# A table of differences made by TensorE, an earlier third weight, and last columns kept by ScalarE

## The reference

```python
# attention, for each step t of S=768 (B=2, H=8, D=40)
m_new = max(f[t] + m, i[t]); fs = exp(f[t] + m - m_new); is_ = exp(i[t] - m_new); m = m_new
C = fs * C + is_ * outer(v[t], k[t]);  n = fs * n + is_ * k[t]
y[t] = sigmoid(o[t]) * (C @ q[t]) / max(|n . q[t]|, 1)
# x: (1536, 320)
xn = x / sqrt(mean(x*x) + 1e-6) * rms_g
x  = (silu(xn @ w_gate) * (xn @ w_val)) @ w_out      # d_ff 1536
h  = x @ w_in;  out = max(0.01 * h, h) @ w_out2      # d_ff 2048
```

## Time and profile before

| what | us |
|---|---|
| median of 3 runs (lowest, highest) | 440.17 (439.88, 440.44) |
| the profiled execution | 440.19 |
| its span, first to last instruction | 438.5 |
| TensorE matmul busy | 429.8 |
| VectorE / ScalarE / GpSimd busy | 226.3 / 193.3 / 91.0 |

### The profile page before, as it was taken

One profiled execution on the slowest core, in us unless ns is written; L12 is line 12 of the kernel. 1 busy time (PEld: TensorE's weight loads), 2 busy tenths in 40 slices (PEclk: granted clock), 3 DMA queues, 4 the chain that ended last, 5 costly groups with the idle time before them and its releaser, 6 DMA issues.

```text
span 438.5 us, 8229 instructions
## 1 busy us (share of the span) xinstructions
PE 429.8 (98%) x3237; PEld 377.7 (86%) x3237; DVE 226.3 (52%) x439; ACT 193.3 (44%) x428; POOL 91.0 (21%) x97
## 2 busy tenths in 40 slices
PE   7999999999999999999999999999999999999997
PEld 5889999999788888878888888989999999999996
DVE  8856656775466555456433335353333333533534
ACT  4867753665262535235333226553343343333332
POOL 1798852212111111002333004430000000000000
PEclk9999999999999999999999999999999999999999
DMA  7887623431202410001222102300000000100101
GB/s 213 279 294 257 215 86 124 126 121 51 78 27 98 131 47 0 1 1 33 66 67 66 34 1 67 100 0 1 0 1 0 1 1 1 44 17 0 61 0 60
DMA packets 10692, 30.42 MB, mean 69 GB/s; under 512 B 1296, under 2 KB 3264, under 8 KB 10656
## 3 DMA queue, kind: packets, MB, share of 16 engines
q1 hardware_dynamic: 10656, 29.92, 21.4%
HBM read 27.90 MB, written 2.01 MB: 68 GB/s over the span
## 4 chain that ended last, share of the span: by engine, by line
PE 82%; issue 6%; POOL 4%; DMA 4%; DVE 3%; ACT 1%; SPq 0%; POOLq 0%; DVEq 0%
PE gate_ps L1166 22%; PE value_ps L1166 22%; PE out_ps L1243 9%; PE out_ps L1205 9%; PE turn_ps L1243 6%; PE out_ps L1209 3%; PE c_ps L1243 3%; PE turn_ps L1131 3%; POOL w_sb L483 2%; DMA raw<-in_w 2%; PE turn_ps L1092 1%; DMA att_sb<-in_tok 1%; PE turn_ps L1109 1%; PE c_ps L1121 1%; DMA y_acc<-in_first_gates 1%
## 5 line engine op out<-in xcount | busy, mean ns | idle before, releaser
L1166 PE MATMUL value_ps<-x_hi,w_sb 128*128 128x512 f32 (+1 forms) x280 | 68.6, 367 | 0.5 <-DVE h_lo L929 0.5
L1166 PE MATMUL gate_ps<-x_hi,w_sb 128*128 128x512 f32 (+1 forms) x280 | 68.8, 368 | 0.2
L1166 PEld LDWEIGHTS gate_ps<-x_hi,w_sb 128*128 128x128 f32 x280 | 47.4, 191 | 8.2 <-DVE x_odd L895 1.1
L1166 PEld LDWEIGHTS value_ps<-x_hi,w_sb 128*128 128x128 f32 x280 | 47.7, 191 | 7.4 <-DVE h_lo L929 0.7
L908 DVE SCALAR_TENSOR_TENSOR act_buf<-act_buf,gate_ps 128x512 f32<-128x512 f32 (+1 forms) x46 | 26.2, 569 | 48.1 <-ACT act_buf L619 47.9
L934 DVE TENSOR_TENSOR h_lo<-hid,h_hi 128x512 fp32r<-128x512 f32 x48 | 33.2, 692 | 33.7 <-ACT h_hi L638 33.7
L633 ACT ACTIVATE h_hi<-value_ps 128x512 fp32r<-128x512 f32 (+1 forms) x46 | 23.0, 500 | 58.4 <-DVE value_ps L915 58.2
L1205 PE MATMUL out_ps<-h_hi,w_sb 128*128 128x512 f32 (+1 forms) x184 | 48.2, 348 | 0.0
L638 ACT ACTIVATE h_hi<-hid 128x512 fp32r<-128x512 f32 x48 | 30.3, 632 | 37.6 <-DVE hid L922 36.5
L619 ACT ACTIVATE act_buf<-gate_ps 128x512 f32<-128x512 f32 (+1 forms) x46 | 23.1, 501 | 49.3 <-PE gate_ps L1166 49.1
L1243 PE MATMUL out_ps<-w_sb,h_hi 128*128 128x320 f32 x192 | 43.0, 309 | 0.2 <-DVE h_lo L934 0.2
(11 more groups left out here) (148 smaller groups left out, 797.5 us busy)
## 6 DMA issues: line engine op xcount, KB each, us to landing
raw<-in_w SPq DMA_DIRECT2D x12, 544.0 KB, 4.6
att_sb<-in_tok SPq DMA_DIRECT2D x12, 484.0 KB, 4.8
raw<-in_w SPq DMA_DIRECT2D x16, 352.0 KB, 3.0
expo<-decay_scratch SPq DMA_DIRECT2D x10, 512.0 KB, 5.3
att_sb<-in_qk SPq DMA_DIRECT2D x24, 160.0 KB
out_y<-y_acc SPq DMA_DIRECT2D x12, 160.0 KB, 1.9
consts_sb<-in_consts SPq DMA_DIRECT2D x1, 129.5 KB, 2.7
y_acc<-in_first_gates SPq DMA_DIRECT2D x1, 112.0 KB, 2.6
```

Source lines behind the costliest of these rows:

```text
L1166: last = nc.tensor.matmul(ps[:, 0:n], lhs, rhs, start=(j == 0), stop=(j == len(xs) - 1))
```

## The change

There are four edits. (1) The later input gates stay as they are; in place of five transposes of the subtracted table TensorE makes ten matmuls that accumulate in pairs, the gates' block against a unit matrix of 16 x 16 and the block of `stab` against the same with -1, which ScalarE writes once into a new tile `minus_unit` from the constants. The subtraction at L968 and the wait for it go. (2) For tile 1 ScalarE, not VectorE, copies the last columns, one half after each of its exponential groups; the semaphore `first_kept` becomes one for each tile. (3) ScalarE rounds weight 2 ahead of `square(0)`, not behind it. (4) SyncE issues the load of weight 2 ahead of its wait for the sums and their store, not behind them.

```diff
--- before.py
+++ after.py
@@ -141,7 +141,9 @@
 
             unit = sb(first, "unit", [P, P], BF16)
             unseen = sb(first, "unseen", [P, P], BF16)
-            used = 4 * (2 * ATT + EXPO * H * P + 2 * H * DV + 6 * DM + 16 + 2 * H + 2 * PAIRS * DV + 3 * TILES * H
+
+            minus_unit = sb(first, "minus_unit", [P, NG])
+            used = 4 * (2 * ATT + EXPO * H * P + 2 * H * DV + 6 * DM + 16 + NG + 2 * H + 2 * PAIRS * DV + 3 * TILES * H
                         + TILES * PAIRS + 3 * H + 8) + 4 * P
             if used < 4 * GF * W2:
                 sb(first, "room", [P, GF * W2 - used // 4])
@@ -225,6 +227,7 @@
         first_gates_in = sem("first_gates_in")
         gates_in = sem("gates_in")
         masks_set = sem("masks_set")
+        minus_set = sem("minus_set")
         rows_set = sem("rows_set")
         consts_in = sem("consts_in")
         cleared = sem("cleared")
@@ -251,7 +254,7 @@
         s_done = sem("s_done")
         p_done = sem("p_done")
 
-        first_kept = sem("first_kept")
+        first_kept = [sem(f"first_kept{n}") for n in range(FIRST)]
         last_done = sem("last_done")
         kw_done = sem("kw_done")
         faded = sem("faded")
@@ -384,9 +387,9 @@
             load_tok(1)
             load_raw(0, W1RAW, w1[0, :, :])
             load_raw(1, W1RAW, w1[1, :, :])
+            load_raw(2, W1RAW, w1[2, :, :])
             sp.wait_ge(a_done, 3)
             sp.dma_start(sums[:, 1:, :], by_time[:, 1:, :]).then_inc(scratch_out, 16)
-            load_raw(2, W1RAW, w1[2, :, :])
             sp.wait_ge(scratch_out, 16)
             load_decays(2)
             load_raw(3, W1RAW, w1[3, :, :])
@@ -458,7 +461,7 @@
 
             def weigh_keys(n):
                 if n < FIRST:
-                    pool.wait_ge(first_kept, 2 * n + 2)
+                    pool.wait_ge(first_kept[n], 2)
                 else:
                     pool.wait_ge(last_done, n - FIRST + 1)
                 pool.wait_ge(tok_in[n % 2], 16 * (n // 2 + 1))
@@ -551,6 +554,12 @@
                     ins = nc.scalar.activation(d, x, ACT.Exp, bias=c_tab[:, n * H + h:n * H + h + 1])
                 ins.then_inc(decay_done, 1)
 
+            def keep_first(n, z):
+
+                act.wait_ge(decay_done, 2 * n + z + 1)
+                w = expo[:, n, :].rearrange("p (h t) -> p h t", h=H)[:, z::2, P - 1:P]
+                nc.scalar.activation(last_decay[:, n, z::2].unsqueeze(2), w, ACT.Copy).then_inc(first_kept[n], 1)
+
             def keep_last(n):
 
                 act.wait_ge(decay_done, 2 * n + 2)
@@ -652,17 +661,21 @@
                     nc.scalar.activation(y_acc[:, c * CHUNK_TILES + k, :], y_ps(c, k)[:, 0:DM], ACT.Copy)\
                         .then_inc(y_evac, 1)
 
+            act.wait_ge(consts_in, 16)
+            nc.scalar.activation(minus_unit[0:NG, :], ident_sb[0:NG, 0:NG], ACT.Copy, scale=-1.0).then_inc(minus_set, 1)
             act.wait_ge(tab_ps, 1)
             nc.scalar.activation(c_tab[:, 0:NG], first_c_ps, ACT.Copy).then_inc(tab_done, 1)
             for n in range(FIRST):
                 for z in range(2):
                     decay(n, z)
+                    if n:
+                        keep_first(n, z)
             ogate(0)
             ogate(1)
             hi_weights(0)
             hi_weights(1)
+            hi_weights(2)
             square(0)
-            hi_weights(2)
             square(1)
             normalise(0)
             normalise(1)
@@ -791,9 +804,11 @@
 
                 if n < FIRST:
                     dve.wait_ge(decay_done, 2 * n + z + 1)
-                    w = expo[:, n, :].rearrange("p (h t) -> p h t", h=H)[:, z::2, P - 1:P]
-                    nc.vector.tensor_copy(last_decay[:, n, z::2].unsqueeze(2), w).then_inc(first_kept, 1)
-                    dve.wait_ge(first_kept, 2 * n + z + 1)
+                    if n == 0:
+
+                        w = expo[:, n, :].rearrange("p (h t) -> p h t", h=H)[:, z::2, P - 1:P]
+                        nc.vector.tensor_copy(last_decay[:, n, z::2].unsqueeze(2), w).then_inc(first_kept[n], 1)
+                    dve.wait_ge(first_kept[n], z + 1)
                 else:
 
                     dve.wait_ge(last_done, n - FIRST + 1)
@@ -965,7 +980,7 @@
             for n in range(FIRST):
                 for z in range(2):
                     scores(n, z)
-            nc.vector.tensor_tensor(ig[0:NG, rest], ig[0:NG, rest], m, ALU.subtract).then_inc(a_done, 1)
+
             for n in range(FIRST):
                 denominator(n)
                 finish(n)
@@ -1057,6 +1072,16 @@
                                                src[0:NG, t * P:(t + 1) * P], ident_sb[0:NG, 0:NG])
                 last.then_inc(tab_ps, 1)
 
+            def difference(ps, a, b, t0, t1):
+
+                pe.wait_ge(minus_set, 1)
+                for t in range(t0, t1):
+                    cols = ps[:, (t - t0) * NG:(t - t0 + 1) * NG]
+                    tok = slice(t * P, (t + 1) * P)
+                    nc.tensor.matmul(cols, a[0:NG, tok], ident_sb[0:NG, 0:NG], start=True, stop=False)
+                    last = nc.tensor.matmul(cols, b[0:NG, tok], minus_unit[0:NG, :], start=False, stop=True)
+                last.then_inc(tab_ps, 1)
+
             def unseen_tokens():
                 pe.wait_ge(masks_set, 2)
                 for n in range(FIRST):
@@ -1263,8 +1288,7 @@
             within(1)
             pe.wait_ge(a_done, 3)
             table(later_a_ps, acum, 1, SEQ_TILES)
-            pe.wait_ge(a_done, 4)
-            table(later_c_ps, ig, 1, SEQ_TILES)
+            difference(later_c_ps, ig, stab, 1, SEQ_TILES)
             update_state(0)
             pe.wait_ge(tab_done, 3)
             nc.tensor.matmul(later_last_ps, last_row_sb, a_tab[:, NG:], start=True, stop=True).then_inc(tab_ps, 1)
```

## The result

The changed kernel takes 443.41 us (median of 17 runs, 440.42 to 445.80) against 440.39 for the kernel before (17 runs, 439.69 to 440.88): a ratio of 1.0065, 95% interval 1.0051 to 1.0079. It is slower by 3 us; 441.0 was predicted, and 442.2 was the end of the range.

What follows compares the result with a forecast made beforehand. TensorE, busy 429.8 of 438.5 us, bounds the kernel, so the feed-forward stream's start sets the end: +1.63 for passes, -0.58 for holes, +1.05; between +0.60 and +1.05 for the clock, +0.83, giving 441.0 us, range 439.8 to 442.2.

Steps and rivals of the forecast that it cites:

- The price of a pass: TensorE's new float32 matmuls, before the first gate product: 0.109 us a pass, 1.63 us added; by the bounds 0.5 to 3.7.
- Two records for one transpose's: On TensorE, a float32 matmul leaves two records and a transpose one, so 20 passes replace 5.
- The holes: TensorE's waits ahead of L1270 and around the turns absorb 0.30 to 0.68 us of the added work; 0.58 taken.
- VectorE's relief: Dropping the subtraction at L968 frees 0.84 us on VectorE from 13.33 to 14.17; value for the kernel: nothing.
- ScalarE's copies and the earlier rounding: Tile 1's last columns on ScalarE (0.4 to 0.6 us more there) and weight 2 rounded before `square(0)`: value nothing.
- The load order: Weight 2's load ahead of the sums' store: weight lands about as before, store at about 15.5 instead of 14.3; value nothing.
- The last rival: Later transfers delay weights near 35 us, 0.28 us of room: +0.3 to +0.8 on top, 441.5 us; chance 0.10.
- The clock: TensorE's rate rise, some 3.2 us into the feed-forward matmuls: keeping its distance costs 1.05 us, keeping its moment 0.60.
- The earlier rise: Rival: new matmuls bring the clock up before the first gate product, giving 439.9 down to 439.3 us; chance 0.07.

Runs made afterwards that it cites:

- halves experiment: The changed kernel with each of the ten matmuls split into two of 64 stationary columns, one to each half of the output's partitions: 440.91 us, ratio 1.0009.
- the kernel without the differences: The changed kernel with the VectorE subtraction at L968, its wait and the five transposes put back, the other three edits kept: 440.75 us, ratio 1.0010.

## Why the prediction was wrong

- **The price of a pass: wrong, and the whole miss.** The prediction took 0.109 us, "the row nearest to the new pass", and kept 0.21 as the upper bound. It measured 0.213, the upper bound. With it the sum is 20 x 0.213 - 0.55 = 3.7 instead of 1.63, and with the same holes the stream starts 3.7 - 0.58 = 3.1 later; 3.28 was measured. That is 2.2 us more than the 1.05 of the forecast, and the end came 2.1 us later than forecast (2.97 against 0.83). "The interval goes with the columns loaded ... and not with the moving ones" was half of a rule. The two rows compared differed in two more things than the columns: the transposes are another kind of operation, and the score-times-value products go to the two halves of the array in turn. At 0.053 us a record, two records a matmul and two halves served in turn, a matmul of 64 columns holds its half for 0.21 us, and one of 128 would take 0.42; 0.43 was measured. The halves experiment is this reading turned round.
- **Two records for one transpose's: right**, 20 records for 5. The count was seen and the weight of each was not.
- **The holes: right in size, not in place.** 0.58 was taken, 0.54 given back (3.81 at tile 0's state products, 3.27 at tile 1's). The 0.30 ahead of L1270 (now L1294) was right; of the rest the prediction had up to 0.26 ahead of the first turn and next to nothing behind it, and the trace has 0.05 ahead of it and 0.19 behind.
- **VectorE's relief worth nothing: right.** The second denominator starts at 15.69, with the end of tile 1's products; c_tab follows the differences at 20.59.
- **ScalarE's copies and the earlier rounding worth nothing: right** (440.43 with both, 440.38 before).
- **The load order worth nothing: wrong by itself, right in the changed kernel as far as the runs tell.** It costs 0.4 alone. The last rival named the place, late weights at 35 us with 0.28 us of room; the store does land later, but that the 0.4 arises there isn't shown. That rival had a later stream and later transfers add up. In the traces with a late stream (halves, the changed kernel) nothing is lost at that place, so they don't add up there.
- **The clock.** The rise neither kept its moment (23.7) nor its distance: the first trace has it 2 to 2.7 us behind the stream's start, a second has an early rise, a fall, and another rise. The earlier rise, given 0.07, did take place in some runs; its gain was mainly the differences' own cost halved, and it ended near before's time, not below it. That the first three runs of before lie within 0.6 us was no sign for the changed kernel. What the clock does between 16 and 19 us matters little where TensorE has holes there: in the kernel without the differences it was high, TensorE waited 0.82 us for VectorE, and the stream started at 20.50. Where the twenty records stand there it matters by more than 2 us (stream at 21.09 or 23.82).

## What to carry to other kernels

A float32 transpose is no measure for a float32 matmul of the same shape: on this trace the matmul costs four times as much, 0.43 against 0.11 us for 128 stationary columns at the low clock. Compare a new matmul with a row of the same kind, type and place in the array, and where rows of two kinds lie a factor of two apart, let the range and the forecast lean to the dearer one. A small subtraction is cheaper left on VectorE, or made behind the transposes, than moved to a TensorE that sets the start of everything else. Where the runs of a kernel fall into two groups, compare their granted clocks before their medians.

## What was not expected of the hardware

- A float32 matmul with 16 rows, 128 stationary and 16 moving columns takes 0.43 us at the low clock, four times a float32 transpose of the same block (0.107) and far more than a bfloat16 matmul of the same shape (0.03). Split into two halves of 64 stationary columns, one on each half of the output's partitions, it costs half (20 records in 4.36 us, 40 in 2.25).
- A busy TensorE alone doesn't settle the clock. In one trace it was busy without a hole from 12 to 16 us, with narrow float32 products, at a granted clock of 0.50; in another the clock rose within the same products (a mean of 0.91 over 14 to 16); in a third it fell from 1.00 to 0.50 between 19 and 20 us, where TensorE had been busy without a hole since 12.19.
- One kernel's runs fell into two groups 2 to 3 us apart with the moment of the clock's rise, at the same stream of instructions.
